# Outputs wait for keys and mask, the last recurrence steps reordered, folds in pieces, and the last MLP column row by row

## The reference

```
y[t]  = r[t] @ (state + (u * k[t]) v[t]^T)
state = w * state + k[t] v[t]^T
```

```
logits = x @ phi
d = softmax of logits over tokens;  slot_input = d.T @ x
slot_out[e] = relu(slot_input[e] @ w1[e]) @ w2[e]
c = softmax of logits over slots;   x = c @ slot_out
```

## Time and profile before

| | us |
|---|---|
| median of 3 runs | 397.99 |
| lowest and highest | 397.24, 398.98 |
| the profiled execution | 398.17 |
| its span in the profile | 396.4 |
| TensorE busy | 387.0 |
| VectorE busy | 243.3 |
| ScalarE busy | 234.7 |
| GpSimd busy | 76.2 |

### The profile page before, as it was taken

The page is one execution under the profiler, slowest core; times in us unless marked ns, Lnnn a source line. Parts: engine busy times, 40 slices in busy tenths (PEclk is TensorE's granted clock), DMA queues, the critical chain, the costliest instruction groups (busy, mean ns, idle before and its releaser), DMA issues.

```text
span 396.4 us, 11104 instructions
## 1 busy us (share of the span) xinstructions
PE 387.0 (98%) x4275; PEld 351.8 (89%) x4275; DVE 243.3 (61%) x415; ACT 234.7 (59%) x617; POOL 76.2 (19%) x93
## 2 busy tenths in 40 slices
PE   8999999999998999999999999999999999999996
PEld 8888989898985444699999999999999999999995
DVE  7886878787735400788656566565565555655553
ACT  5565667666653244877565655655655655655662
POOL 7466777677411000000000000000000000000000
PEclk9999999999999999999999999999999999999999
DMA  7999999997899999300010010010100100100101
GB/s 176 335 271 244 264 263 256 278 295 191 262 408 410 428 416 414 136 2 0 2 60 2 0 62 1 18 44 2 60 0 0 60 1 0 60 2 0 60 2 60
DMA packets 15087, 54.92 MB, mean 139 GB/s; under 512 B 2512, under 2 KB 5968, under 8 KB 13776
## 3 DMA queue, kind: packets, MB, share of 16 engines
q1 hardware_dynamic: 14496, 54.47, 42.2%
q10 hardware_dynamic: 560, 0.05, 0.1%
HBM read 49.79 MB, written 4.72 MB: 138 GB/s over the span
## 4 chain that ended last, share of the span: by engine, by line
PE 97%; ACT 1%; issue 1%; DVE 1%; ACTq 0%; POOL 0%; POOLq 0%
PE ps L1136 17%; PE ps L1141 17%; PE ps L1137 17%; PE ps L865 7%; PE ps L1114 6%; PE ps L910 5%; PE ps L904 5%; PE ps L889 3%; PE ps L878 3%; PE ps L1065 3%; PE ps L1046 3%; PE ps L944 3%; PE ps L923 2%; PE ps L932 1%; PE ps L1006 1%; PE ps L1054 1%
## 5 line engine op out<-in xcount | busy, mean ns | idle before, releaser
L1136 PE MATMUL ps<-w_hi,g_hi 128*128 128x384 f32 x384 | 130.5, 340 | 0.0
L1137 PE MATMUL ps<-w_lo,g_hi 128*128 128x384 f32 x384 | 129.5, 337 | 0.0
L652 DVE SCALAR_TENSOR_TENSOR g_full<-h_full 128x384 f32<-128x384 f32 x128 | 71.4, 558 | 84.4 <-ACT h_full L827 84.0
L838 ACT ACTIVATE g_hi<-g_full 128x384 fp32r<-128x384 f32 x128 | 67.2, 525 | 73.6 <-DVE g_full L652 73.3
L1141 PE MATMUL ps<-w_hi,g_lo 128*128 128x384 f32 x384 | 88.7, 339 | 0.0
L1136 PEld LDWEIGHTS ps<-w_hi,g_hi 128*128 128x128 f32 x384 | 72.0, 187 | 0.5 <-issue 0.5
L1137 PEld LDWEIGHTS ps<-w_lo,g_hi 128*128 128x128 f32 x384 | 72.1, 188 | 0.0
L641 DVE TENSOR_TENSOR g_lo<-g_full,g_hi 128x384 fp32r<-128x384 f32 x128 | 70.6, 552 | 0.7 <-ACT g_hi L838 0.6
L1141 PEld LDWEIGHTS ps<-w_hi,g_lo 128*128 128x128 f32 x384 | 69.2, 188 | 0.0
L827 ACT ACTIVATE h_full<-ps 128x384 f32<-128x384 f32 x128 | 62.3, 487 | 9.7 <-PE ps L1114 0.6
L734 ACT ACTIVATE bonus_v<-nat,bonus 128x48 f32<-128x48 f32 x192 | 45.9, 322 | 0.8
(11 more groups left out here) (130 smaller groups left out, 357.0 us busy)
## 6 DMA issues: line engine op xcount, KB each, us to landing
rk<-rk_t SPq DMA_DIRECT2D x48, 192.0 KB, 4.4
nat<-rkv SPq DMA_DIRECT2D x21, 384.0 KB, 6.4
w_units<-late_units SPq DMA_DIRECT2D x5, 1536.0 KB, 14.1
w_units<-late_units SPq DMA_DIRECT2D x8, 768.0 KB, 7.4
x_unit<-late_units SPq DMA_DIRECT2D x3, 1536.0 KB, 13.0
out<-y_out SPq DMA_DIRECT2D x7, 576.0 KB, 3.0
m_unit<-late_units SPq DMA_DIRECT2D x2, 1536.0 KB, 11.5
w_units<-w_in SPq DMA_DIRECT2D x4, 768.0 KB, 17.3
```

What stands on the lines that cost most here:

```text
L652: dve.scalar_tensor_tensor(out=g_full[:, f % 2], in0=h_full[:, f % 2], scalar=0.01, in1=h_full[:, f % 2], op0=ALU.mult, op1=ALU.max).then_ ...
L838: act.activation(g_hi[:, f % 4], g_full[:, f % 2], ACT.Copy).then_inc(g_hi_done, 1)
L1136: pe.matmul(bank, g_hi[:, f % 4, bass.ts(s, P)], w_hi[:, f], start=(f == 0), stop=False)
L1137: pe.matmul(bank, g_hi[:, f % 4, bass.ts(s, P)], w_lo[:, f], start=False, stop=False)
```

## The change

The following are changed: outputs() waits for the tile's load (kv_loaded) in place of bonus_v_done; outputs(0) stands ahead of sum_bonus(1). The last two steps leave the loop: outputs(23) stands ahead of turn_x(22), turn_x(23) uses a bank of its own (BANK_S), three of the ones go, ScalarE copies both x_t before both x. The last chunk's maximum is taken from PSUM, and the last transpose of logits stands behind the product that spreads the row maximum; the subtractions wait for logits one chunk at a time. Both folds are done in pieces: groups_in in two, slot_in_t in three, groups_out in two, slot_out_t in three (VectorE, ScalarE, VectorE), each piece with a bank of its own. The transposes of softmax group 4 stand behind the first product of slot_w_in; the copies of groups 3, 4 and 5 move one place later. In the last column of the last block the nine products are ordered by row, and each row has its semaphore. WARM goes from 22 to 19.

```
     BUFS = 4
-    WARM = 22
+    WARM = 19
     POWERS_MADE = 10
...
         BANK_S, BANK_Y, BANK_D, BANK_T = 0, 4, 6, 7
+        LAST_TURN = BANK_S
+        IN_BANKS, OUT_BANKS = (3, 5, 6), (7, 3, 4)
...
                     12: (14, 1), 13: (15, 1)}
-        turned_at = {6: 0, 8: 1, 11: 2, 12: 3}
+        turned_at = {2: (4, 0), 3: (4, 1), 5: (4, 2), 6: (4, 3), 8: (5, 0), 9: (5, 1), 11: (5, 2), 12: (5, 3)}
...
-            chunk_maximum(C - 1)
+            dve.wait_ge(logits_t_ready, C)
+            dve.tensor_reduce(chunk_max[:, C - 1:C], ps[:, BANK_T, DM:DM + P], AX.X, ALU.max).then_inc(chunk_done, 1)
             dve.wait_ge(chunk_done, C)
...
             dve.wait_ge(mx, 2)
-            dve.wait_ge(logits_kept, C + 1)
             for n in range(C):
+                dve.wait_ge(logits_kept, n + 2)
                 dve.tensor_tensor(dispatch[:, bass.ts(n, 4)], logits[:, bass.ts(n, 4)],
...
             dve.wait_ge(disp_ready, 3)
-            dve.tensor_copy(groups_in[:], ps[:, 2, 0:XW]).then_inc(groups_copied, 1)
-            dve.wait_ge(slot_in_turned, 1)
-            dve.tensor_copy(slot_in_t[:], ps[:, 3, 0:KT * SL].rearrange("p (k s) -> p k s", s=SL)).then_inc(slot_in_ready, 1)
+            dve.tensor_copy(groups_in[:, 0:P], ps[:, 2, 0:P]).then_inc(groups_copied, 1)
+            dve.tensor_copy(groups_in[:, P:XW], ps[:, 2, P:XW]).then_inc(groups_copied, 1)
+            for kt in range(KT):
+                dve.wait_ge(slot_in_turned, kt + 1)
+                dve.tensor_copy(slot_in_t[:, kt], ps[:, IN_BANKS[kt], 0:SL]).then_inc(slot_in_ready, 1)
...
             dve.tensor_tensor(combine2[:, :, 1], combine[:], combine2[:, :, 0], ALU.subtract).then_inc(cmb, 1)
-            dve.wait_ge(so_turned, 1)
-            dve.tensor_copy(slot_out_t[:], ps[:, 7, 0:KT * P].rearrange("p (k s) -> p k s", s=P)).then_inc(so_ready, 1)
+            for kt in (0, 2):
+                dve.wait_ge(so_turned, kt + 1)
+                dve.tensor_copy(slot_out_t[:, kt], ps[:, OUT_BANKS[kt], 0:P]).then_inc(so_ready, 1)
...
-            dve.wait_ge(g_used, FFT * N_BLOCKS)
+            dve.wait_ge(last_summed[1], 1)
             dve.wait_ge(out_stored[1], 16 * (N_BLOCKS // 2 - 1))
...
                 if c >= 1:
-                    act.wait_ge(chunk_done, c)
+                    act.wait_ge(chunk_done, c if c < C - 1 else C)
                 act.activation(chunk_logits_t[:], ps[:, BANK_T, DM:DM + P], ACT.Copy).then_inc(logits_t_kept, 1)
...
                 act.wait_ge(x_turned, j + 1)
-                act.activation(x_t[:, j % B].rearrange("p k t -> p (k t)"), ps[:, BANK_T, 0:DM], ACT.Copy).then_inc(xt_copied, 1)
+                bank = LAST_TURN if j == STEPS - 1 else BANK_T
+                act.activation(x_t[:, j % B].rearrange("p k t -> p (k t)"), ps[:, bank, 0:DM], ACT.Copy).then_inc(xt_copied, 1)
...
                     copy_xt(i - 2)
+                if 2 <= i < STEPS:
                     copy_x(i - 2)
...
                     scale_v(i)
+            copy_x(STEPS - 2)
+            copy_x(STEPS - 1)
             keep_logits_t(C - 1)
...
             act.wait_ge(w2_done, E)
-            act.activation(groups_out[:], ps[:, 4, 0:DM], ACT.Copy, scale=slot_scale[:, 1:2]).then_inc(so_copied, 1)
+            act.activation(groups_out[:, 0:P], ps[:, 4, 0:P], ACT.Copy, scale=slot_scale[:, 1:2]).then_inc(so_copied, 1)
+            act.activation(groups_out[:, P:DM], ps[:, 4, P:DM], ACT.Copy, scale=slot_scale[:, 1:2]).then_inc(so_copied, 1)
+            act.wait_ge(so_turned, 2)
+            act.activation(slot_out_t[:, 1], ps[:, OUT_BANKS[1], 0:P], ACT.Copy).then_inc(so_ready_act, 1)
...
+            high_swin(1, 2, 0, P)
             act.wait_ge(cmb_turned, 5)
-            copy_softmax(3)
-            high_swin(1, 2, 0, P)
             high_w_out(0, 1)
-            copy_softmax(4, (0, 1))
+            copy_softmax(3, (0, 1))
             high_swin(2, 5, P, BANK - P)
...
                         if first and odd == 0 and f in turned_at:
-                            copy_softmax(5, (turned_at[f],))
+                            copy_softmax(turned_at[f][0], (turned_at[f][1],))
...
                         if first and k == 0:
-                            copy_softmax(4, (2, 3))
+                            copy_softmax(3, (2, 3))
                         if f == 3 and not (first and odd == 0):
...
-            act.wait_ge(g_used, FFT * N_BLOCKS)
             act.wait_ge(out_stored[1], 16 * (N_BLOCKS // 2 - 1))
             for s in (0, 2):
+                act.wait_ge(last_summed[s], 1)
                 act.activation(y_out[:, 1, s], ps[:, 5 + s, 0:DM], ACT.Copy).then_inc(last_copied[s], 1)
...
-            def turn_x(j, s, c):
+            def turn_x(j, s, c, bank=BANK_T):
                 pe.wait_ge(x_done, j + 1)
-                pe.wait_ge(xt_copied, j + 1)
+                if bank == BANK_T:
+                    pe.wait_ge(xt_copied, j + 1)
                 if s == 0:
...
                 for kt in range(KT):
-                    last = pe.transpose(ps[:, BANK_T, bass.ts(kt, P)], x_step[:, s % 2, bass.ts(kt, P)], ident[:])
+                    last = pe.transpose(ps[:, bank, bass.ts(kt, P)], x_step[:, s % 2, bass.ts(kt, P)], ident[:])
                 last.then_inc(x_turned, 1)
...
-            def outputs(j, s, carried):
+            def outputs(j, s, carried, loads):
...
                 pe.wait_ge(bonus_kept, j + 1)
-                pe.wait_ge(bonus_v_done, j + 1)
+                pe.wait_ge(kv_loaded[s], 16 * loads)
                 if carried:
...
             sum_bonus(0, 0)
-            ones(3, BANK_Y + 1)
+            ones(2, BANK_Y + 1)
+            outputs(0, 0, False, 1)
             sum_bonus(1, 1)
-            outputs(0, 0, False)
             pe.wait_ge(s_clear, 1)
...
                     sum_bonus(i, s)
-                    outputs(i - 1, (n + 1) % B, True)
+                    outputs(i - 1, (n + 1) % B, True, c + 1 + (n + 1) // B)
                     update(i - 1, (n + 1) % B)
...
-            for i in range(B * (C - 1) + 2, STEPS + 2):
-                if i < STEPS:
-                    score(i, i % B)
-                else:
-                    ones(2, BANK_D)
+            for i in range(B * (C - 1) + 2, STEPS):
+                score(i, i % B)
                 turn_x(i - 2, i - 2 - LAST_STATE, C - 1)
-                if i < STEPS:
-                    sum_bonus(i, i % B)
-                if i <= STEPS:
-                    outputs(i - 1, (i - 1) % B, True)
-                else:
-                    ones(2, BANK_D)
+                sum_bonus(i, i % B)
+                outputs(i - 1, (i - 1) % B, True, 1 + (i - 1) // B)
                 if i == LAST_STATE + 2:
                     turn_logits(LAST_STATE + 2, C)
+            outputs(STEPS - 1, B - 1, True, C)
+            turn_x(STEPS - 2, B - 2, C - 1)
+            ones(1, BANK_D)
+            turn_x(STEPS - 1, B - 1, C - 1, LAST_TURN)
+            ones(2, BANK_D)
             logits_t(C - 1)
-            ones(2, BANK_D)
-            turn_logits(STEPS + 1, C + 1)
             ones(2, BANK_D)
...
             pe.matmul(ps[:, 1, 0:P], row_max[:].to_broadcast([P, P]), ident[:], start=True, stop=True).then_inc(mx_pe, 1)
+            turn_logits(STEPS + 1, C + 1)
             pe.wait_ge(s_pad, 10)
...
                     last.then_inc(disp_ready, 1)
-            pe.wait_ge(groups_copied, 1)
             for kt in range(KT):
-                last = pe.matmul(ps[:, 3, bass.ts(kt, SL)], groups_in[:, bass.ts(kt, P)], fold[:, 0:SL], start=True, stop=True)
-            last.then_inc(slot_in_turned, 1)
+                pe.wait_ge(groups_copied, min(kt + 1, 2))
+                pe.matmul(ps[:, IN_BANKS[kt], 0:SL], groups_in[:, bass.ts(kt, P)], fold[:, 0:SL], start=True, stop=True)\
+                    .then_inc(slot_in_turned, 1)
             pe.matmul(ps[:, 4, 0:1], fold[:], groups_in[:, DM:XW], start=True, stop=True).then_inc(scale_sum, 1)
...
-            pe.wait_ge(slot_in_ready, 1)
             def unit_parts(n):
...
                     for kt in range(KT):
+                        if e == 0:
+                            pe.wait_ge(slot_in_ready, kt + 1)
                         for j in range(GROUPS):
...
             turn_softmax(3)
-            pe.wait_ge(so_copied, 1)
             for kt in range(KT):
-                last = pe.matmul(ps[:, 7, bass.ts(kt, P)], groups_out[:, bass.ts(kt, P)], fold[:], start=True, stop=True)
-            last.then_inc(so_turned, 1)
-            turn_softmax(4)
-            pe.wait_ge(so_ready, 1)
+                pe.wait_ge(so_copied, min(kt + 1, 2))
+                pe.matmul(ps[:, OUT_BANKS[kt], 0:P], groups_out[:, bass.ts(kt, P)], fold[:], start=True, stop=True)\
+                    .then_inc(so_turned, 1)
             pe.wait_ge(win_loaded[0], 16)
             for kt in range(KT):
+                if kt == 1:
+                    pe.wait_ge(so_ready_act, 1)
+                else:
+                    pe.wait_ge(so_ready, 1 + kt // 2)
```

(10 more changed lines are left out.)

2 lines of the change are left out of this document (added).

## The result

The changed kernel takes 395.87 us (median of 11 runs, 394.39 to 399.46) beside 398.14 (396.67 to 398.98) of the kernel before: ratio 0.9956, 95% interval 0.9935 to 0.9977. The forecast was 396.4, in a range of 394.7 to 397.8. So the sum came out, but as will be seen several of its terms did not.

A forecast was written before the change was run, and what follows sets the result against it. TensorE's queue was taken as the bound, with saturated transfers fixing landings in the first recurrence steps and from 102 us on. Gains 0.4 + 0.25 + 0.9 = 1.55 us took 398.17 to 396.6, 396.4 as median; range 394.7 to 397.8.

The forecast's parts named there:

- Start: First recurrence steps: TensorE reaches score(3) 1.9 us earlier, but score(4) waits for step 4's rk tile; 0.4 us kept.
- End of the recurrence: Last steps through the row maximum: fewer ones, reordered outputs and transpose shorten TensorE's path to the experts by 1.6 us.
- Fold before the experts: Copying groups_in in pieces lets products start sooner, about 1.35 us instead of 1.82: gain 0.45 us.
- Fold behind: From groups_out to the second slot product, pieces on two engines take about 2.05 us instead of 3.15: gain 1.1.
- what is late next: MLP start: w_out's first quarter holds ScalarE's split, so of TensorE's lead there only 0.25 us is kept, bounds 0 to 0.8.
- The landing: w_out's first quarter: its load moves only with the recurrence's 0.4 us, releasing ScalarE's split at 158.8 us.
- Softmax parts in f = 2, 3, 5, 6: Moved ScalarE copies, 0.37 us each, cost nothing under TensorE's ten products; uncovered they would cost 1.5 us.
- Last column: End of the kernel: row-by-row sums let the stores leave earlier, gain 0.9 us, bounds 0.5 and 1.0.
- A: Transfers are not the bound; landings follow their issue or the rings have slack: 393.5 us, chance 10%.
- B: Step 4's rk tile lands sooner, so 1.9 us of the start is kept and the weight stream moves: 394.9 us, 15%.
- C: The start and the MLP keep nothing and only the last column pays: 397.1 us, chance 10%.
- D: TensorE's idle gap before the MLP drops its clock to the lower level, costing 2.7 us: 399.1 us, chance 7%.

The follow-up runs named there:

- experiment 3: The changed kernel, unchanged, run and profiled a second time, with the kernel before also repeated: 396.41 us, ratio 0.9964 to the kernel before.
- experiment 1: Changed kernel with the softmax copies of f = 5 and f = 9 moved ahead of the quarter's split on ScalarE: 395.04 us, ratio 0.9916 to the kernel before.
- experiment 2: Changed kernel with w_out's first quarter sent ahead of the last two quarters of w_in: 395.07 us, ratio 0.9908 to the kernel before.
- experiment 4: Changed kernel with both the two softmax copies moved ahead and w_out's first quarter sent earlier: 394.38 us, ratio 0.988 to the kernel before.
- experiment 11: Changed kernel with the 1.5 MB load of unit 1 moved behind the first rk tiles, in two halves: 398.68 us, ratio 0.9985 to the kernel before.
- experiment 6: Changed kernel with the old start put back, including outputs waiting for the bonus: 396.53 us, ratio 0.995 to the kernel before.
- experiment 7: Kernel before with only the end of the recurrence changed, outputs still waiting for the bonus: 398.47 against 398.66 us, ratio 0.999.
- experiment 10: Changed kernel with two softmax copies moved ahead, w_out's first quarter sent earlier and the old start put back: 395.86 us, ratio 0.9936 to the kernel before.
- experiment 8: Kernel before with the recurrence's end changed and w_out's first quarter sent ahead of w_in's last two: 397.67 us, ratio 0.998.
- experiment 9: Kernel before with only w_out's first quarter sent ahead of w_in's last two quarters: 398.35 us, ratio 1.0002.
- experiment 5: Kernel before with only the last column's products ordered row by row: 397.82 against 398.22 us, ratio 0.9992.

## Why the prediction was right, and where it was not

**Start, 0.4 forecast, 0.46 found, by luck.** In the changed kernel's profile score(4) began 0.92 us later than before, not 0.4 earlier; the 0.46 come from the stalls of the kernel before at 34.78 and 35.59, which the changed kernel did not have. The bound is there: in 11 of the 14 profiles the scaling of step 4 begins within 0.03 us of its tile's landing, at 23.1 to 24.8. But the way to it was shorter than I had it. I forecast score(3) 1.9 us earlier and then 1.5 us of idle time. It began at 19.68, 20.21 and 20.24 in experiments 3, 1 and 2, 0.8 to 1.35 earlier than in the kernel before, at 21.55 in experiment 4 and at 21.89 in the changed kernel's profile; idle time of 1.5 us in front of score(4) is in none. The lead was there at score(2) (14.66 to 15.34, where the old start has 16.12 to 16.99), and the stall near 18 us, which only the new start has, took the rest. Experiment 11, in which the tile was there at 19.70, began score(4) only 0.08 us before experiment 3: TensorE's own queue, stalls included, ends almost as late as the tile. And score(23) spreads from 107.92 to 110.27 over five profiles with the new start (without experiment 11's) and from 108.48 to 110.17 over eight with the old one: the landing itself moves, and TensorE's stalls are longer in one execution and shorter in the next. The means differ by 0.5 us; single profiles say nothing about a term of this size.

**End of the recurrence, 1.6 forecast, 1.99 found.** The step was right and 0.4 small. Some 0.2 of the difference is chance: the section holds a stall of 0.46 us before and of 0.25 in the changed kernel (in experiment 11, which has none there, it took 10.31). The part behind logits_t gave 0.45 (2.10 to 1.65) where I had 0.6. What the forecast did not see is in experiments 6, 7 and 10: 0.88 of it come from the wait for the bonus, of which I had said that in the loop it is long met. It is met in the old order; in the new order the last outputs would stand behind bonus_v, whose 1.92 us are then on the chain.

**Fold before the experts, 0.45 forecast, 0.38 found.** Right.

**Fold behind, 1.1 forecast, and behind it "what is late next".** Here lie the forecast's errors. The fold itself was worth half: from groups_out to the product that was at 158.51 there are 2.59 us in the chain of experiment 2 instead of 3.15, since the turn of the softmax (L1038, 0.22) stands in it now and the fold's products last longer. Then I took ScalarE's 0.18 us before w_hi as the sign that w_out bounds the MLP and kept 0.25. Experiments 8 and 9 show that it bounded nothing then: the chain of before stays on TensorE past it. In the four profiles in which the landing did hold the first product of g_hi back (experiments 1, 3 and 11, and the changed kernel itself, just), this product came 3.47 to 3.49 us after w_hi; before, it came 163.72 - 159.22 = 4.50 after, so w_hi had 1.0 us of slack, an estimate from these profiles. In the new order it has until 7.79 - 3.49 = 4.30 us behind groups_out without delaying this product, and 4.29 is where it came (in experiment 6 it came at 4.21, and the product at 7.79 again).

**The landing, 158.8 forecast, 156.74 found.** Two things moved it. The first of its 16 completions came at 154.76 instead of 155.52: 0.76, where I had 0.4. The last came 1.98 us after the first instead of 3.67: 1.69. The first part is more than the recurrence's share: the stream did not run independently of TensorE, as I had assumed. In experiment 5 a stall delayed the last outputs, and the load that waits for them was issued at 115.80 instead of 114.67; the DMA share at 118 to 122 us (second last number) fell under 1, and the first completion came at 156.46, 0.94 later than before, although score(23) was 0.96 earlier. Experiment 5, then the kernel before:

```profile
118.00:120.00 2.00, 1.98 (x32) 1.74 (x29) 0.56 (x1) 0.06 (x1) 0.00 (x0) 1.00 0.78 264
...
118.00:120.00 2.00, 1.85 (x33) 1.41 (x32) 0.17 (x1) 0.90 (x2) 0.00 (x0) 1.00 1.05 401
```

The second part is not shown to be an effect of the change: this spread is 2.4 to 3.6 in the other profiles of the changed kernel and of the edits that leave the stream alone, 3.2 to 3.7 in the three of kernels with the old recurrence's end and the old stream, and 2.3 in experiment 7. So the profiled execution had a fortunate landing, at the edge of the slack; experiment 1, with 157.66, shows the other case: 1.6 us more to the first product of g_hi. At 158.8, 2.1 later than found, the loss would have been some 2 us, an estimate from these two profiles.

**Softmax parts in f = 2, 3, 5, 6, "nothing" forecast, 0.9 found** (experiment 1), together with those of f = 8 and 9. The cover that I named, ten products of TensorE, is there for most f. It is not there where ScalarE first waits for a quarter's product; the copy behind that wait adds to a chain of four dependent steps. The uncovered 1.5 us was the right bound and the wrong value.

**Last column, 0.9 forecast, 0.96 found**, 0.97 alone.

The sum: forecast 0.4 + 0.25 + 0.9 = 1.55; found 0.46 + 1.99 + 0.38 - 0.31 - 0.88 + 0.96 - 0.02 = 2.58 in the profiles (the spans differ by 2.59), 2.3 and 1.4 us in the medians of the two sets of runs, and 1.8 and 1.4 by their ratios (0.9956 and 0.9964). I let the MLP keep 0.65 us of TensorE's lead, and it kept 1.64: the landing came 2.1 us earlier than forecast, and the copies took 0.9 of that back. The forecast time was met because these errors offset one another, and that is luck. Of my own signs of being wrong two came true: w_out's quarter landed before 158 us, and the clock was granted under 1. Of the signs of being right, the dispatch products and groups_out came 2.45 and 2.83 us earlier (2.0 and 2.4 forecast), ScalarE waited for the quarter's DMA and the third store left at once; the idle time of TensorE before score(4) and before the first g_hi product was not there.

**Rivals.** A (nothing bound by transfers) is out: w_hi waited for its DMA. B needed the tile of step 4 early; it was at 23.73. C is out by the MLP's share of 1.64. D, the clock: it did fall, at 19.13 for 3.41 us, not at the MLP, and not after a wait for data but 0.1 us behind the end of the stall of 1.26 us. That cost the scaling 0.8 us (24.54 behind the landing at 23.73), not the 2.7 I had priced. In the gap before the MLP it stayed at 1.00: the idle time of 2.3 us that I forecast for TensorE there isn't in the changed kernel, and in experiment 11, where ScalarE waits 3.98 us, TensorE has 1.40 us of it and keeps its clock. The Trainium skill ("TensorE: Matmul & The Clock Gate", "Loop structure matters more than you think") holds that long waits between bursts of matmuls bring the clock down. The fall behind the stall of 1.26 us agrees with that, though the wait was short; the 1.40 us at the MLP did not bring it down.

## What to carry to other kernels

Idle time that ends with a DMA on a side engine is no bound yet: follow the released instruction to the product that needs it, and subtract. When a small copy is moved on a side engine, look at which wait it stands behind, not at how much time the engine has over; behind a wait for the main engine it lengthens the whole dependent chain. And a wait that is always met can become the last one when the work behind it is moved forward. Last, a section that comes out as forecast is no proof of its term: look at the steps inside it, as the start shows here.
